# Two runs of twelve projection matmuls a step instead of four of six, with the products in another order around them

## The reference

```python
def _moe_ref(x, w1, w2, w3, w_out):
    h = np.maximum(np.maximum(x @ w1, x @ w2), x @ w3)
    return (h @ w_out).astype(np.float32)

def _moe2_ref(x, w_in, w_out):       # x: 4608 x 512, w_in: 512 x 2048, w_out: 2048 x 512
    h = x @ w_in
    g = h - np.tanh(h)
    return (g @ w_out).astype(np.float32)
```

## Time and profile before

| | us |
|---|---|
| median of 3 runs | 1443.42 |
| lowest, highest | 1443.27, 1444.77 |
| the profiled execution, its own time | 1445.15 |
| its span in the profile | 1443.4 |
| TensorE busy (10776 matmuls) | 1428.4 (99% of the span) |
| VectorE busy | 1005.8 (70%) |
| ScalarE busy | 642.8 (45%) |
| DMA engines, mean busy share | 53% |

### The profile page before, as it was taken

How to read it: one execution, slowest core, us unless ns; L and a number is a source line. 1 busy time by engine, 2 the same in 40 slices (tenths; PEclk the granted TensorE clock), 3 DMA queues, 4 the chain that set the end, 5 groups by cost and what they waited for, 6 DMA issues and landing times.

```text
span 1443.4 us, 26250 instructions
## 1 busy us (share of the span) xinstructions
PE 1428.4 (99%) x10776; PEld 1237.4 (86%) x10776; DVE 1005.8 (70%) x1781; ACT 642.8 (45%) x1275; POOL 94.6 (7%) x140
## 2 busy tenths in 40 slices
PE   8999999999999999999899999999999999999998
PEld 7988888888888878788788999999999998999997
DVE  6886666666666655535787777777777777777776
ACT  3322222222222222224565666566566565666654
POOL 2402121212121100000000000000000000000000
PEclk9999999999999999999999999999999999999999
DMA  9244444444443211156877676676766667676551
GB/s 343 80 158 156 152 158 150 156 152 142 166 143 119 107 70 41 71 191 239 300 253 252 220 245 226 205 254 216 255 219 237 225 212 253 218 253 221 190 179 49
DMA packets 78743, 269.74 MB, mean 187 GB/s; under 512 B 6880, under 2 KB 21216, under 8 KB 66976
## 3 DMA queue, kind: packets, MB, share of 16 engines
q1 hardware_dynamic: 78624, 268.07, 53.2%
HBM read 210.89 MB, written 57.15 MB: 186 GB/s over the span
## 4 chain that ended last, share of the span: by engine, by line
PE 95%; DVE 2%; DMA 1%; ACT 1%; issue 0%; SPq 0%; DVEq 0%; ACTq 0%
PE psum L657 30%; PE psum L697 26%; PE psum L722 25%; PE psum L671 10%; PE psum L600 2%; PE psum L640 2%; DMA x_scratch<-x_stage 1%; DMA k_first<-in_k 0%; DVE probs L1023 0%; DVE probs L1005 0%; DVE k_pooled L984 0%; DVE row_max L1001 0%; DVE g L1091 0%; DVE poly L1112 0%; DVE turned L1028 0%
## 5 line engine op out<-in xcount | busy, mean ns | idle before, releaser
L657 PE MATMUL psum<-x,w 128*128 128x512 f32 (+1 forms) x2160 | 454.0, 371 | 1.3 <-DVE x L1034 1.0
L657 PEld LDWEIGHTS psum<-x,w 128*128 128x128 f32 x2160 | 377.8, 190 | 72.0 <-issue 2.1
L697 PE MATMUL psum<-w_out_s,g 128*128 128x512 f32 x1680 | 433.3, 393 | 0.5 <-DVE g L1091 0.4
L697 PEld LDWEIGHTS psum<-w_out_s,g 128*128 128x128 f32 x1680 | 298.4, 189 | 50.6 <-DVE g L1091 1.3
L722 PEld LDWEIGHTS psum<-x_even,ring 128*128 128x128 f32 x1680 | 223.4, 192 | 18.0 <-ACT copies L864 5.0
L722 PE MATMUL psum<-x_even,ring 128*128 128x256 f32 x1680 | 227.5, 283 | 4.6 <-ACT copies L864 4.6
L1096 DVE SCALAR_TENSOR_TENSOR poly<-poly,u_sq 128x512 f32<-128x512 f32 x144 | 99.5, 691 | 173.8 <-ACT poly L861 173.8
L722 PEld LDWEIGHTS psum<-x_odd,ring 128*128 128x128 f32 x1344 | 178.0, 191 | 10.9 <-DMA x_odd<-x_scratch 0.4
L722 PE MATMUL psum<-x_odd,ring 128*128 128x256 f32 x1344 | 181.3, 283 | 0.0
L864 ACT ACTIVATE copies<-psum 128x256 f32<-128x256 f32 x288 | 101.5, 377 | 171.6 <-PE psum L722 171.6
L818 ACT ACTIVATE h<-best 128x512 fp32r<-128x512 f32 (+1 forms) x60 | 35.4, 589 | 270.3 <-DVE best L1049 270.3
(11 more groups left out here) (80 smaller groups left out, 1011.1 us busy)
## 6 DMA issues: line engine op xcount, KB each, us to landing
ring<-w_scratch SPq DMA_DIRECT2D x72, 1024.0 KB, 5.0
ring<-w_scratch SPq DMA_DIRECT2D x72, 768.0 KB, 4.4
x_scratch<-x_stage SPq DMA_DIRECT2D x18, 1792.0 KB, 6.1
x_odd<-x_scratch SPq DMA_DIRECT2D x28, 512.0 KB, 5.7
x_even<-x_scratch SPq DMA_DIRECT2D x28, 512.0 KB, 5.5
w_scratch<-w_stage SPq DMA_DIRECT2D x32, 384.0 KB, 2.6
v_raw<-in_v SPq DMA_DIRECT2D x21, 512.0 KB, 4.4
q_t<-in_q SPq DMA_DIRECT2D x36, 256.0 KB, 3.9
```

What stands on the lines that cost most here:

```text
L657: mm = pe.matmul(psum[:, bank, 0:hi - lo], w123[:, m, ws, n, c, :], x[:, xs, c, lo:hi], start=(c == 0 and ws + xs == 0), stop=(c == KC1 - ...
L697: mm = pe.matmul(psum[:, j, :], g_of(c)[:, gs, j * P:(j + 1) * P], w_out_s[:, row_of(c), ws, :], start=(m == 0 and gs + ws == 0), stop=(m ...
```

## The change

A step of stage 2 has two places for the projection in place of four, with all twelve matmuls of a chunk at each. In steps 0 to 2 the layer-2 work stands in two pieces of nine matmuls in place of three of six. Product 3 is now issued ahead of product 2, so two counts of `multiplied` move: ScalarE's copy after product 3 waits for three products and not four, VectorE's `sum_first` for four and not three. SyncE's waits (four products, seven products) keep their numbers; the fourth product is now product 2.

```diff
                 if s < EARLY:
-                    if n < 3:
-                        layer2(("l2", NT - 1, C_ORDER[s + 1]), range(2 * n, 2 * n + 2))
+                    layer2(("l2", NT - 1, C_ORDER[s + 1]), range(3 * n, 3 * n + 3))
                 else:
-                    project(2 * (s - 2) + n // 2, (0, 1) if n % 2 == 0 else (2, 3))
+                    project(2 * (s - 2) + n, range(SUB))
...
                 multiply(1, second, True, False)
+                between(s, 0)
+                pe.wait_ge(copied, 5 * s + 1)
+                multiply(3, main, False, False)
                 if s >= 1:
                     pe.wait_ge(summed, 3 * s - 1)
                 multiply(2, third, True, True)
-                between(s, 0)
-                pe.wait_ge(copied, 5 * s + 1)
-                multiply(3, main, False, False)
                 pe.wait_ge(w_in_half[p % 2][1], 16 * loads)
                 pe.wait_ge(copied, 5 * s + 2)
                 multiply(4, second, False, True)
-                between(s, 1)
                 pe.wait_ge(copied, 5 * s + 3)
                 multiply(5, main, False, False)
-                between(s, 2)
+                between(s, 1)
                 pe.wait_ge(copied, 5 * s + 4)
                 multiply(6, main, False, True)
-                between(s, 3)
...
-                act.wait_ge(multiplied, PRODUCTS * s + 4)
+                act.wait_ge(multiplied, PRODUCTS * s + 3)
                 copy_sum(s, 1)
...
             def sum_first(s):
-                dve.wait_ge(multiplied, PRODUCTS * s + 3)
+                dve.wait_ge(multiplied, PRODUCTS * s + 4)
```

## The result

The changed kernel takes 1454.95 us (median of 6 runs, 1452.73 to 1456.56), the kernel before 1444.84 (median of 6, 1443.27 to 1445.74): a ratio of 1.0067, 95% interval 1.0057 to 1.0078, slower by 10.1 us where 8.4 was forecast. The profiled span went from 1443.4 to 1452.1, by 8.7.

A forecast was written before the change was run, and what follows sets the result against it. The prediction took stage 2 to be bound by TensorE's instruction stream; -2.6 + 9.6 + 1.4 - 0.7 + 0.7 = +8.4 us, added to the median 1443.42, gave 1451.8 us, range 1448.0 to 1456.0.

The forecast's parts named there:

- The seams: Stage 2, steps 3 to 71: fewer switches between products and projections, 0.04 us less in about 65 steps, -2.6 us.
- The rival that they cost nothing: Changes between products and projections in stage 2 cost no time, the rest as forecast: 1454.4 us; 8 in 100.
- (a): Step 2 of tiles 1 to 8: first projection waits for the late bank drain, 1.2 us a tile, +9.6 us.
- (b): Last x2 load of tile 1, issued in step 7 behind the ring load: 1.36 later, TensorE waits, +1.4 us.
- (c): Step 4's wait for the last x2 store: landing taken at 708.6, less of the step left after it, -0.7 us.
- (d): Last projections of step 71 wait for g, whose chain starts 0.68 later with the last sum: +0.7 us.
- Steps 0 to 2: First steps of stage 2, with layer-2 pieces of nine matmuls: claimed to gain next to nothing.
- The clock did not fall at the drains: Rival: every drain wait at a new tile brings TensorE to 1.2 GHz, +12 us, 1464; 4 in 100.
- short wait: Rival: in every step, at product 5 or sum_first's successors, 0.1 us by 69, 1459 us; 6 in 100.

The follow-up runs named there:

- product 2 back: The change with product 2 put back ahead of the first projection of a step: 1450.07 us, ratio 1.0044 to the kernel before.

## Why the prediction held, and where it didn't

- **The seams, -2.6.** Right: 10.52 a step, 2.52 us over 63 steps. The lengths of two kinds of run gave the price of a seam to a few nanoseconds. The rival that they cost nothing is out (662.76 against 665.28). That its time, 1454.4, is nearer to the measured 1454.95 than mine is luck: the gap comes from the base and the spread of executions, told under the sum.
- **(a) The drains, +9.6.** Right, and shown by removal: 9.98 us. The wait was 1.04 us and the slower start behind it 0.2, for 1.1 and 0.1. That two drains are late and not one was in the prediction's times, but not drawn from them. ScalarE's wait hid VectorE's, and taking the first away bought 1.7 us of the 10.
- **(b) The x2 load, +1.4.** Right: +1.26 with three steps' seams in it, so 1.38 for the load; the wait in front of step 8 is 1.35 us, where some 1.6 was named. Issued first, it takes away 1.51 in the change and 0.13 in the kernel before (31.81 to 31.68). Those 0.13 are a third place where TensorE waited before, which the prediction's opening left out and this term had.
- **(c) Steps 3 and 4, -0.7.** -1.08 was measured. The landing was put at 708.6, the middle of two bounds, which is a weak reason; 708.5 was luck in part, since the other kernels show the landing to hang on the order of the ring load and the store. The prediction counted it from an unmoved T0 of step 3. From the T0 that there was, it came 0.44 earlier, and that is the difference of nearly 0.4. The clock cost 1.6 us here and had cost 1.5, as assumed; with the same code and the same wait it cost 2.4 in another run (5.29 for 2.87), so this too could have come out otherwise.
- **(d) The end, +0.7.** Right: +0.66. The last sum of step 71 starts 9.18 us after its T0 before and 9.86 in the change, 0.68 later, and so do the last projections. With product 2 back it is another 0.70 later and the end takes 0.69 more.
- **Steps 0 to 2, next to nothing.** They took 0.20 to 0.25 more in every kernel with the new pieces, and 32.95 in both with the old. Most of it lies in step 2, where the run of 24 products takes 3.06 us (681.93 to 684.99) for 2.87:

```profile
681.93 3.21 PE L721 MATMUL psum<-x_even,ring 128*128 128x256 f32 x24
683.75 0.37 ACT L861 ACTIVATE copies<-psum 128x256 f32<-128x256 f32 x1
```

  ScalarE's copy of product 3 ends at 684.12. Product 5 could start at 684.09, 0.12 behind the last matmul of product 4; its first matmul comes 0.09 late and the second another 0.10. In this step ScalarE has a copy of stage 1's sums to make as well. The prediction looked for this wait in ordinary steps, where the copy has 0.8 us to spare, and not in this one. That the extra copy is the cause is argued; no run took it out.
- **The sum.** 8.4 for 8.7 in the span, in part because misses cancel: +0.35 up to T0 of step 3 and +0.4 of the drains stand against -0.4 of (c). The forecast of 1451.8 was 3.2 below the median of 1454.95. Of that, 1.4 is the base: the median of three runs, 1443.42, on which I put the sum, became 1444.84 with six. 0.3 is the terms. The rest, 1.5, lies between spans and medians: the profiled execution of the change took 1453.8, 1.15 below its median, that of before 1445.15, 0.3 above. Executions differ by as much before stage 2 starts: T0 of step 0 lies between 658.3 and 661.6 in nine profiles.
- **The rivals.** The clock did not fall at the drains (1.00 through the 1.03 us wait at 775 us). No short wait came up in every step of the change itself; it did in "product 2 back", at product 5, the place the prediction named.

## What to carry to other kernels

When a stream is reordered, look for what was queued behind the moved piece on the other engines, and measure its slack against the rarest step, not the ordinary one: here an ordinary step had 0.8 us or more to spare, and eight of the 72 lacked 1. A copy whose input has long been ready was best placed at the head of its engine's step, not behind a chain that it doesn't need. And a wait that vanishes uncovers the next in line; all that depend on the same late event have to be moved together.

## What the runs showed of the hardware

- A run of projections (128 x 512) after products (128 x 256) takes 1.39 us for the first six matmuls and 0.2267 each from there on; with two changes of shape there and back fewer, a step took 0.040 us less, 0.02 for each.
- After a wait of 1.03 us the run of twelve took 0.06 longer than 2.75, and the seam itself 0.15 more than the wait.
- Behind an idle stretch of 3.6 us (708.0 to 711.6) the granted clock was 0.59 from 711.6 to 715.0; through one of 1.0 us it was 1.00 (775.0 to 778.5). After almost the same idle stretch (3.57 and 3.54 us) the clock over the next 24 matmuls was 0.62 in one kernel and 0.50 in another with the same code there, 0.84 us apart.
- The time of a DRAM store of 1792 KB from issue to landing was 6.8 to 10.9 us with the order and spacing of one 1024 KB load and the store, in the same crowded 10 us.
